# An expert's third weight chunk is split by VectorE ahead of the expert instead of inside it, and GpSimd instead of SyncE waits for the last scatters

## The reference

```python
expert_idx = np.argmax(x @ w_gate, axis=1)          # 1536 tokens, 8 experts
# up to 384 tokens of an expert are gathered into disp[e]
h = np.maximum(np.einsum('ecd,edf->ecf', disp, w1), 0.0)   # 384 -> 1024
y = np.einsum('ecf,efd->ecd', h, w2)                       # 1024 -> 384
out[i] = gate_w[i] * y[expert_idx[i], pos[i]]
```

## Time and profile before

| what | value |
|---|---|
| median of 3 runs | 466.21 us |
| lowest and highest | 464.45 and 467.45 us |
| the profiled execution | 464.45 us |
| its span, first to last instruction | 462.6 us |
| mean granted TensorE clock | 0.991 |
| PE, DVE, ACT, POOL busy | 440.2, 313.0, 251.2, 50.1 us |

### The profile page before, as it was taken

The page is one execution under the profiler, slowest core; times in us unless marked ns, Lnnn a source line. Parts: engine busy times, 40 slices in busy tenths (PEclk is TensorE's granted clock), DMA queues, the critical chain, the costliest instruction groups (busy, mean ns, idle before and its releaser), DMA issues.

```text
span 462.6 us, 15102 instructions
## 1 busy us (share of the span) xinstructions
PE 440.2 (95%) x6263; PEld 418.3 (90%) x6263; DVE 313.0 (68%) x786; ACT 251.2 (54%) x515; POOL 50.1 (11%) x64
## 2 busy tenths in 40 slices
PE   4799999999999999999999999999999898999995
PEld 3688999999999999999999999989998778999994
DVE  4988955867677877687867638655555977678510
ACT  1265765446544663565355566563457875677421
POOL 6000000000000100010000100221020332221201
PEclk9999999999999999999999999997999999999999
DMA  7718976760310023000000166522765998620001
GB/s 259 279 65 258 322 247 238 279 256 4 124 68 3 36 84 110 1 20 21 3 1 4 37 249 231 172 85 74 277 198 197 308 365 254 216 62 3 30 1 45
DMA packets 35645, 63.44 MB, mean 137 GB/s; under 512 B 3980, under 2 KB 21950, under 8 KB 35568
## 3 DMA queue, kind: packets, MB, share of 16 engines
q1 hardware_dynamic: 33264, 57.88, 37.1%
q0 software_dynamic: 2304, 4.47, 2.6%
HBM read 50.77 MB, written 14.19 MB: 140 GB/s over the span
## 4 chain that ended last, share of the span: by engine, by line
PE 85%; DVE 8%; issue 3%; ACT 1%; DMA 1%; POOLq 0%; SPq 0%; DVEq 0%; ACTq 0%
PE bank L683 21%; PE bank L669 20%; PE pair L588 6%; PE bank L885 6%; PE bank L838 5%; PE pair L550 3%; PE bank L892 3%; PE pair L838 3%; PE pair L853 3%; PE bank L853 3%; DVE KRW L1153 2%; DVE AD L1172 2%; PE pair L609 2%; PE pair L644 1%; PE pair L885 1%
## 5 line engine op out<-in xcount | busy, mean ns | idle before, releaser
L669 PE MATMUL bank<-XH,W 128*128 128x256 f32 x576 | 119.1, 283 | 0.0
L683 PE MATMUL bank<-W,GH 128*128 128x384 f32 x372 | 98.9, 347 | 0.0
L669 PEld LDWEIGHTS bank<-XH,W 128*128 128x128 f32 x576 | 94.6, 188 | 0.7
L669 PE MATMUL bank<-XL,W 128*128 128x256 f32 x288 | 80.5, 280 | 0.0
L1018 ACT ACTIVATE RB<-bank 128x256 f32<-128x256 f32 x96 | 36.7, 382 | 55.8 <-PE bank L669 55.2
L683 PEld LDWEIGHTS bank<-W,GH 128*128 128x128 f32 x372 | 62.0, 188 | 1.3
L683 PE MATMUL bank<-W,GL 128*128 128x384 f32 x186 | 62.7, 337 | 0.0
L1209 DVE TENSOR_TENSOR GL<-GG,GH 128x256 fp32r<-128x256 f32 x96 | 40.4, 421 | 29.1 <-ACT GH L924 28.6
L924 ACT ACTIVATE GH<-GG 128x256 fp32r<-128x256 f32 x96 | 40.1, 418 | 36.1 <-PE bank L683 34.4
L588 PE MATMUL pair<-KRW 48*64 48x32 f32 (+1 forms) x2304 | 46.1, 228 | 10.8 <-DMA KRW<-in_krw 5.6
L588 PEld LDWEIGHTS pair<-KRW 48*64 48x64 f32 (+1 forms) x2304 | 40.4, 142 | 17.6 <-DVE KRW L1154 6.8
(11 more groups left out here) (162 smaller groups left out, 688.4 us busy)
## 6 DMA issues: line engine op xcount, KB each, us to landing
raw<-in_moe_w SPq DMA_DIRECT2D x23, 768.0 KB, 7.3
stage<-in_moe_w SPq DMA_DIRECT2D x9, 768.0 KB, 8.1
KRW<-in_krw SPq DMA_DIRECT2D x12, 512.0 KB, 6.0
slots<-X SPq DMA_DIRECT2D x8, 579.0 KB, 5.8
VV<-in_v SPq DMA_DIRECT2D x12, 288.0 KB, 6.9
KRW<-in_krw SPq DMA_DIRECT2D x12, 256.0 KB, 6.3
stage<-in_moe_w_in SPq DMA_DIRECT2D x4, 768.0 KB, 7.1
stage<-in_moe_w_out SPq DMA_DIRECT2D x4, 768.0 KB, 7.1
```

The costliest lines, as they stand in the source:

```text
L669: last = nc.tensor.matmul(bank[4 + f % 2][:, 0:2 * P], win[wa][:, c, f * P:(f + 1) * P], xa[:, c, :], start=n == 0, stop=n == 3 * KM - 1)
L683: last = nc.tensor.matmul(bank[6 + m][:, 0:DM], ga[(NF * g + f) % G3][:, cols], wout[wa][:, f, :], start=f == 0 and n == 0, stop=f == NF - ...
```

## The change

On DVE the low part of chunk 2 of expert e + 1 is now made behind that of chunk 1 at the end of expert e. Inside an expert chunk 2 is split only for e = 0. On POOL the waits for the scatters and the increments of `yo_free` are now done for the last expert too, and the final three waits stand at POOL's end instead of SP's.

```diff
@@ block.sync
                 for c in range(CH):
                     load_part(n + c)
-            for m in range(MT):
-                sp.wait_ge(scat2[m], 16 * NE)
@@ block.gpsimd
-                if e < NE - 1:
-                    for m in range(MT):
-                        pool.wait_ge(scat2[m], 16 * (e + 1))
-                        pool.sem_inc(yo_free[m], 1)
+                for m in range(MT):
+                    pool.wait_ge(scat2[m], 16 * (e + 1))
+                    pool.sem_inc(yo_free[m], 1)
+
+            for m in range(MT):
+                pool.wait_ge(scat2[m], 16 * NE)
@@ block.vector, hidden_low
-                    if f == 2:
-                        split_low_expert(e, CH - 2)
+                    if f == 2 and e == 0:
+                        split_low_expert(0, CH - 2)
                     if f == 4:
                         split_low_expert(e, CH - 1)
 
             def hidden_low_small(e, m, high, ready):
+                if m == 0 and e == 0:
+                    split_low_expert(0, CH - 2)
                 if m == 0:
-                    for x in (CH - 2, CH - 1):
-                        split_low_expert(e, x)
+                    split_low_expert(e, CH - 1)
@@ the loop over experts
                     split_low_expert(e + 1, 1)
+                    split_low_expert(e + 1, 2)
```

## The result

The changed kernel takes 468.95 us (median of 9 runs, 467.79 to 470.28) against 466.2 us for the kernel before (9 runs, 464.45 to 467.49). The ratio is 1.0064 with a 95% interval of 1.0042 to 1.0086: 3.0 us more, 2.0 to 4.0. The forecast was 467.1 us in a range of 464.0 to 470.4, that is +0.9 us. So the direction and the size class (within 1%) came out, and some two thirds of the cost were not in the sum. The time lies in the range because the range had been drawn around the rivals: rival 1 in its smaller reading, with expert 6, gives 466.2 + 0.9 + 1.9 = 469.0 us.

What follows compares the result with a forecast made beforehand. PE was taken as the bound, busy 95% of 462.6 us. On the runs' median of 466.21 us, +0.9 (expert 6) and 0 (end) gave 467.1 us, range 464.0 to 470.4.

Steps and rivals of the forecast that it cites:

- rival 1: Program end: POOL's DRAIN is paid in full behind the landing, +3.1 us, or +1.9 in its smaller reading; chance 0.25.
- The bound, and small experts: PE bounds and never waits for low parts in large experts; DVE's work order in experts 1, 2, 3, 5 unchanged: 0.
- Large experts 4, 6, 7: One DVE split moves ahead of block 0: 0 in 4 and 7 (idle time), +0.9 us in 6 (PE stops before block 3).
- The loads: Loads set off by splits: only chunk 29's moves, starting 4.17 us earlier, and its landing does not matter: 0.
- The waits at the end: Final scatter waits move from SP to POOL; its DRAIN starts about 461.3 but still ends at 462.4: 0, range -0.9 to +3.1.
- the one to which it gave 0.4: The forecast case: PE stops in expert 6, +0.9 us, and the program's end stays where it is; chance 0.4.
- Rival 2: Program end: POOL's DRAIN collapses once the scatter has landed, -0.9 us, cancelling expert 6, 466.2 us; chance 0.15.
- Rival 3: PE's gaps before experts 3 and 4 change: closing gives 464.0 us, growing 470.2 us; chance 0.1, half each way.

Runs made afterwards that it cites:

- pool_only: The change's edits on SP and POOL alone, DVE's order as in the kernel before: 467.51 us, ratio 1.0030 against the kernel before.
- drains_inside: Kernel before plus four POOL DRAINs: one ahead of its first scatter, two behind its last into the slots, one behind expert 5's landed scatters; 464.03 us, ratio 0.9958.
- the two halves: Against the kernel before: the DVE move alone, 467.07 us (ratio 1.0020), and the SP and POOL edits alone, 467.51 us (ratio 1.0030).
- drain_behind_6: Kernel before with one more DRAIN on POOL, behind the landed scatters of expert 6: 465.00 us, ratio 0.9976 against the kernel before.

## Why the prediction was right and wrong

**The bound, and small experts.** Right. PE without a stop in the large experts was the reason for the value 0 of all that the move gives back, and no kernel with the move was faster than its counterpart without it.

**Large experts 4, 6, 7.** Right in place and size: 0, +0.9 and 0 were given; the profile after has 0, +0.94 and 0. For expert 4 the 0 was partly luck. Taking the split away from expert 6 alone removes the stop, putting it behind block 0 shortens it, doing it twice adds the second one in full, 1.76 us. What the step did not see is how thin the cover of expert 4 is. Its 1.58 us of idle time on DVE come from the same slow passage at the branch that holds PE up, so they are not a property of the kernel; in two executions with a short gap (0.56 and 1.01 us) expert 4 stopped as well.

**The loads.** Right. Chunk 29's load goes from 389.35 to about 385.6, and nothing waits for it.

**The waits at the end.** This is the step that failed. The prediction took 0, because "a DRAIN that outlasts the landing by 1.6 us is most simply read as bound to the scatter's own bookkeeping". The DRAIN does go by the number of scatters, but what it waits for does not run on by itself: behind a landed scatter it takes 3.005 us, and with a memset in between it still ends 3.01 us behind the memset. What POOL does in this time no trace shows. Queued behind the landing, it is paid in full. That is rival 1 in its smaller reading, priced at +1.9 us; the profile after has +1.8, pool_only +1.4 (0.5 to 2.4). The start at 461.3, with 0.45 us for queue instructions behind the landing, was sized nearly right: the DRAIN of the changed kernel starts at 462.93, 0.36 us behind the landing at 462.56. So the outcome was the case to which the prediction gave 0.25, and the one to which it gave 0.4 had the end wrong. The rule of the Trainium skill that stood against the row (VectorE: DVE Perf Modes, section "The DRAIN you can't avoid") has some 12 ns on every engine for the DRAINs of the preamble and postamble. The trace comes near it for POOL only where POOL had issued no scatter since the last DRAIN: 41 and 46 ns in drains_inside. With 3 to 36 scatters it was 0.29 to 3.0 us. On the other engines the DRAIN on L58 took 7 ns (SP, before) and 122 ns (SP, after), and in the changed kernel 514 ns (DVE), 449 ns (ACT) and 3.098 us (PE). So the figure fits SP's at best, and whether the page means this DRAIN is open.

**Rivals 2 and 3.** Rival 2's short DRAIN fell with pool_only. Rival 3's gaps do vary, between executions of the same order of work, but no more with the move than without it; and the sum of the two halves, 0.9 + 1.4 = 2.3 us, agrees with the 3.0 us (2.0 to 4.0) of the whole change without them. That the gaps are fetches of code slowed by full DMA engines was only argued; no run tested it.

**A version that beats both.** Nothing in the move on DVE can gain here, since PE has no gap inside the experts. The end can: drain_behind_6 takes 465.0 us, 0.24% under the kernel before and the first to beat it by design; drains_inside, with more DRAINs, 464.03 us. Their intervals overlap. By the profiles the earlier end of the last DRAIN explains 1.3 of the 2.0 us of drains_inside (0.29 instead of 1.56 us behind the landing); whether its other DRAINs add to that stays open. With the inner DRAIN the last one ends 0.16 us behind the landing in drain_behind_6 (462.02 against 461.86) instead of 1.56, so little more is to be had from it.

## What to carry to other kernels

When an engine's idle time is to take work that is moved, ask what makes it idle: time that comes from another engine's lateness varies with it, and in the one expert where that engine was late already, 1.66 us moved ahead of the first block cost 0.9 us. And do not let the engine that issues software DMAs be the last to wait for them: its closing DRAIN took longer the more of them it had issued, so let another engine wait for the landing while it runs, and put a DRAIN into a pause shortly before the end.

## What was not expected of the hardware

A DRAIN on POOL takes time in proportion to the scatters (indirect DMAs of 128 rows) that POOL has issued since its last DRAIN, also when all of them have landed long ago. The durations where all had landed, over the kernels of this study:

| scatters since the last DRAIN | DRAIN, us |
|---|---|
| 3 | 0.293 |
| 15 | 1.272 |
| 18 | 1.517 |
| 21 | 1.780 |
| 33 | 2.760 |
| 36 | 3.005 |

The slope from first to last is (3.005 - 0.293) / 33 = 0.082 us a scatter, and the rest for none is 0.05 us, which the DRAINs of 41 and 46 ns confirm. Scatters of empty tiles count in full: of the 18 of experts 0 to 5 nine belong to tiles without a token, the three of expert 7 all to tiles with tokens, and one costs (1.517 - 0.05) / 18 = 0.081 us in the one case and (0.293 - 0.05) / 3 = 0.081 in the other.

A DRAIN that starts before the last scatter has landed costs less behind the landing, but goes by their number too:

| scatters since the last DRAIN | kernel | end behind the last landing, us |
|---|---|---|
| 3 | drain_behind_6, at the end | 0.16 |
| 6 | drains_inside, at the end | 0.29 |
| 12 | drains_inside, from 316.8 | 0.54 |
| 36 | before, at the end | 1.56 |

The first three give some 0.04 us a scatter, half of what the queued DRAIN costs, and a line through them gives 1.53 us at 36. Counted from the end of the last scatter's record, the DRAIN of 36 takes the same 3.0 us as the queued one; which of the two readings is the right one these runs do not tell. Whether other software DMAs than these cost the same was not tried.
